# A fused attention and expert kernel: decay inverses by a backward scan, and one product as three products of high and low parts

## What is computed

```python
# r, k, v, w: (4, 8, 768, 48); u: (8, 48)
for t in range(S):                       # per batch and head
    y[t] = r[t] @ (state + outer(u * k[t], v[t]))
    state = w[t][:, None] * state + outer(k[t], v[t])
x = y as (3072, 384)
x = ((x @ w1) * (x @ w2)) @ w3 @ w_out   # w1, w2: 384x1024; w3: 1024x1024; w_out: 1024x384
# then a router (w_gate, w_noise, both 384x8) picks 2 of 8 experts for each token
out = sum over the two of weight * relu(x @ ew1[e]) @ ew2[e]
```

## Time and profile before

| | us |
|---|---|
| median of 3 runs | 982.52 |
| lowest and highest | 981.27, 983.54 |
| profiled execution, its own time | 980.96 |
| its span, first to last instruction | 979.2 |
| PE busy | 947.8 (97%) |
| DVE busy | 676.2 (69%) |
| ACT busy | 528.0 (54%) |
| L263, reciprocals, busy | 82.2 |

### The profile page before, as it was taken

The page is one execution under the profiler, slowest core; times in us unless marked ns, Lnnn a source line. Parts: engine busy times, 40 slices in busy tenths (PEclk is TensorE's granted clock), DMA queues, the critical chain, the costliest instruction groups (busy, mean ns, idle before and its releaser), DMA issues.

```text
span 979.2 us, 18038 instructions
## 1 busy us (share of the span) xinstructions
PE 947.8 (97%) x6825; PEld 894.3 (91%) x6825; DVE 676.2 (69%) x1133; ACT 528.0 (54%) x986; POOL 222.8 (23%) x209
## 2 busy tenths in 40 slices
PE   6989999999999999999989999999999999999995
PEld 4656999999999999999989999999999999999995
DVE  6997769888888875437766765757767468565570
ACT  4454445454555544326545665756657467565560
POOL 0000000202020111021453233333243332334321
PEclk9999999999999999999999999999999999999998
DMA  9996343544445121126557887877968779787751
GB/s 346 302 320 184 115 142 116 160 150 129 134 143 163 50 71 38 51 67 234 188 161 191 237 278 233 250 235 220 307 205 247 254 207 292 218 242 256 200 156 17
DMA packets 94347, 183.74 MB, mean 188 GB/s; under 512 B 18274, under 2 KB 49764, under 8 KB 94260
## 3 DMA queue, kind: packets, MB, share of 16 engines
q1 hardware_dynamic: 80884, 161.90, 50.8%
q0 software_dynamic: 12976, 20.66, 10.2%
q10 hardware_dynamic: 400, 0.02, 0.0%
HBM read 156.94 MB, written 26.97 MB: 188 GB/s over the span
## 4 chain that ended last, share of the span: by engine, by line
PE 87%; DVE 5%; ACT 3%; issue 2%; DMA 1%; SPq 0%; another core or an unknown queue 0%; POOL 0%; DVEq 0%; ACTq 0%; POOLq 0%
PE pp L1231 20%; PE bank L1215 20%; PE bank L786 13%; PE bank L803 7%; PE fx L786 6%; PE fx L803 4%; PE yu L1274 3%; PE pp L184 3%; PE tr L1196 2%; PE yu L1256 1%; PE fx L1256 1%; PE yu L205 1%; PE yu L235 1%; PE tr L193 1%; DVE kdiv L263 1%
## 5 line engine op out<-in xcount | busy, mean ns | idle before, releaser
L1125 POOL DMA_INDIRECT result<-x2s,who x55 | 92.5, 1681 | 290.3 <-ACT x2s L1348 277.4
L1335 DVE SCALAR_TENSOR_TENSOR abl<-bank,abh 128x512 fp32r<-128x512 f32 x96 | 66.2, 691 | 113.7 <-ACT abh L1330 97.5
L976 POOL DMA_INDIRECT slot_entry<-entry,slot_i x48 | 52.1, 1086 | 334.7 <-DVE token_f L965 322.5
L1215 PE MATMUL bank<-xh,set_up_h 128*128 128x256 f32 x384 | 109.2, 284 | 0.0
L1215 PE MATMUL bank<-xh,set_up_l 128*128 128x256 f32 x384 | 108.6, 283 | 0.0
L1215 PE MATMUL bank<-xl,set_up_h 128*128 128x256 f32 x384 | 108.6, 283 | 0.0
L1330 ACT ACTIVATE abh<-bank 128x512 fp32r<-128x512 f32 x96 | 57.5, 599 | 85.1 <-PE bank L1215 79.6
L786 PE MATMUL bank<-xh,w12h 128*128 128x384 f32 x264 | 89.5, 339 | 1.0 <-DVE xl L483 0.9
L786 PE MATMUL bank<-xh,w12l 128*128 128x384 f32 x264 | 88.4, 335 | 0.0
L786 PE MATMUL bank<-xl,w12h 128*128 128x384 f32 x264 | 88.2, 334 | 0.0
L1231 PE MATMUL pp<-set_down_h,abh 128*128 128x384 f32 x256 | 87.7, 342 | 0.0
(11 more groups left out here) (254 smaller groups left out, 2641.4 us busy)
## 6 DMA issues: line engine op xcount, KB each, us to landing
up_raw<-in_moe_w SPq DMA_DIRECT2D x93, 512.0 KB
down_raw<-in_moe_w SPq DMA_DIRECT2D x124, 384.0 KB
wt<-in_w SPq DMA_DIRECT2D x16, 384.0 KB, 3.2
kt<-in_k SPq DMA_DIRECT2D x16, 384.0 KB, 3.1
rt<-in_r SPq DMA_DIRECT2D x16, 384.0 KB, 3.6
vs<-in_v_rows SPq DMA_DIRECT2D x16, 384.0 KB, 3.7
kn<-in_k_rows SPq DMA_DIRECT2D x16, 288.0 KB, 3.2
rn<-in_r_rows SPq DMA_DIRECT2D x16, 288.0 KB, 3.6
```

The source lines that it names most:

```text
L976: nc.gpsimd.indirect_dma_start(slot_entry, bass.IndirectOffsetOnAxis(slot_i[:, s, n:n + 1], 0), entry[:, s, n, :], None).then_inc(scattere ...
L1125: nc.gpsimd.indirect_dma_start(out, bass.IndirectOffsetOnAxis(who[v % 4][:, s, 0:1], 0), yo[v % 2][:, s, 0:DM], None, bounds_check=N - 1, ...
L1215: last = nc.tensor.matmul(bank[m % 2][:, f * T2:(f + 1) * T2], wp[:, kk, c:c + P], xp[:, kk, :], start=(n == 0), stop=(n == 3 * KD - 1))
L1335: nc.vector.scalar_tensor_tensor(hl[:, 2 * m:2 * m + 2, :].rearrange("p a t -> p (a t)"), bank[m % 2][:, :], 0.0, hh[:, 2 * m:2 * m + 2, : ...
```

## The change

The inverse is made backward: one reciprocal of the last element of each of six chunks, then six scans over 127 elements from the end, each multiplying by the decay of the element behind. The load of the decays' input for the pair after next waits for these scans, since they read it, and SP issues it at derive 3, not 0.

Each product of w3 by the output weights becomes three float32r products. ACT makes the high parts (`woh` in two halves after wo_turn 2 and 5, its gate columns at gates_turn; `w3h` of block q + 1 at w3_mm q.1), DVE the low parts (`wol` at wo_gates and gates_turn, `w3l` of block q + 1 at w3_mm q.2), which overwrite the raw values. PE waits for `w3l_ready` where it waited for the load.

```diff
@@ sp_input_load
-            need(sp, (decay_ready, kdiv_ready, rdec_ready)[n], g - 1)
+            need(sp, (inverse_ready, kdiv_ready, rdec_ready)[n], (4, 1, 1)[n] * (g - 1))
@@ dve_inverse
-            two = slice(2 * third, 2 * third + 2)
-            nc.vector.reciprocal(kdiv[q % 2][:, :].rearrange("p (c x) -> p c x", c=NC)[:, two, :],
-                                 decay[q % 2][:, two, 1:C + 1]).then_inc(inverse_ready, 1)
+                nc.vector.reciprocal(kdiv[q % 2][:, :].rearrange("p (c x) -> p c x", c=NC)[:, :, C - 1:C],
+                                     decay[q % 2][:, :, C:C + 1]).then_inc(inverse_ready, 1)
+                dve.wait_ge(inverse_ready, 4 * g + 1)
+            for c in (2 * third, 2 * third + 1):
+                first, end = c * C, (c + 1) * C - 1
+                last = nc.vector.tensor_tensor_scan(backwards(kdiv[q % 2], first, end), backwards(wt[q % 2], first + 1, end + 1),
+                                                    backwards(wt[q % 2], first + 1, end + 1), kdiv[q % 2][:, end:end + 1],
+                                                    ALU.mult, ALU.bypass)
+            last.then_inc(inverse_ready, 1)
@@ sp_attention
-            elif step == "derive" and n in (0, 4, 5):
-                sp_input_load(sp, *after, max(0, n - 3))
+            elif step == "derive" and n >= 3:
+                sp_input_load(sp, *after, n - 3)
@@ first_act
+                def high(q):
+                    act.wait_ge(w3_loaded[q % 2], 16 * (q // 2 + 1))
+                    need(act, wa_full, q - 1)
+                    nc.scalar.copy(w3h[q % 2][:, :, :], w3T[q % 2][:, :, :]).then_inc(w3h_ready, 1)
...
                         evacuate(q)
+                        if q % KD == KD - 1:
+                            four = slice(4 * (q // KD), 4 * (q // KD) + 4)
+                            act.wait_ge(wo_loaded[q // KD], 16)
+                            nc.scalar.copy(woh[:, four, 0:DM], wo[:, four, 0:DM]).then_inc(woh_ready, 1)
...
+                        high(0)
+                    elif step == "gates_turn":
+                        act.wait_ge(gates_full, 2)
+                        nc.scalar.copy(woh[:, :, DM:WA].rearrange("p (j t) e -> p t j e", t=2), gate_columns).then_inc(woh_ready, 1)
+                    if step == "w3_mm" and n == 1 and q + 1 < KF:
+                        high(q + 1)
@@ first_dve
+                def lower_w3(q):
+                    dve.wait_ge(w3h_ready, q + 1)
+                    nc.vector.tensor_tensor(w3l[q % 2][:, :, :], w3T[q % 2][:, :, :], w3h[q % 2][:, :, :].bitcast(f32),
+                                            ALU.subtract).then_inc(w3l_ready, 1)
...
+                    if step == "wo_gates":
+                        for part in range(2):
+                            four = slice(4 * part, 4 * part + 4)
+                            dve.wait_ge(woh_ready, part + 1)
+                            dve.wait_ge(wb_full, KD * (part + 1))
+                            nc.vector.tensor_tensor(wol[:, four, 0:DM], wo[:, four, 0:DM], woh[:, four, 0:DM].bitcast(f32),
+                                                    ALU.subtract).then_inc(wo_ready, 1)
+                    elif step == "gates_turn":
+                        dve.wait_ge(woh_ready, 3)
+                        nc.vector.tensor_tensor(wol[:, :, DM:WA].rearrange("p (j t) e -> p t j e", t=2), gate_columns,
+                                                woh[:, :, DM:WA].rearrange("p (j t) e -> p t j e", t=2).bitcast(f32),
+                                                ALU.subtract).then_inc(wo_ready, 1)
+                        lower_w3(0)
+                    if step == "w3_mm" and n == 2 and q + 1 < KF:
+                        lower_w3(q + 1)
@@ first_pe
-                            pe.wait_ge(w3_loaded[q % 2], 16 * (q // 2 + 1))
-                            pe.wait_ge(wo_ready, 1)
+                            pe.wait_ge(w3l_ready, q + 1)
+                            pe.wait_ge(wo_ready, 3)
...
+                            for part, (wp, op) in enumerate(((w3h[q % 2], woh[:, m, :]), (w3h[q % 2], wol[:, m, :]),
+                                                             (w3l[q % 2], woh[:, m, :]))):
+                                last = nc.tensor.matmul(sums[q % 2][:, 0:WA], wp[:, m, :], op,
+                                                        start=(m == 0 and part == 0), stop=(m == KF - 1 and part == 2))
```

More of the change, by code:

```diff
@@ L254, in dve_decays, with backwards @@
             last.then_inc(decay_ready, 1)
+        def backwards(tile, first, end):
+            whole = tile[:, first:end]
+            (step, rows), _ = whole.ap
+            return bass.AP(whole.tensor, whole.offset + end - first - 1, [[step, rows], [-1, end - first]])
         def dve_inverse(dve, b, q, third):
@@ L502, in program @@
             gates_side = nc.alloc_sbuf_tensor_at("gates_side", [P, 2 * P], f32, offset=token_base + 4 * KD * F1)
+            w3_base = (nc.sbuf_base + 31) // 32 * 32
             w3T = [psb(f"w3T{i}", [P, KF, P]) for i in range(2)]
+            w3l = [nc.alloc_sbuf_tensor_at(f"w3l{i}", [P, KF, P], f32r, offset=w3_base + 4 * KF * P * i) for i in range(2)]
+            w3h = [nc.alloc_sbuf_tensor_at(f"w3h{i}", [P, KF, P], f32r, offset=token_base + 8 * TT * DM + 4 * KF * P * i) for i in range(2)]
+            woh = psb("woh", [P, KF, WA], f32r)
             pads = psb("pads", [P, PADS, WORDS], i32)
@@ L588, in first_act @@
                         nc.scalar.copy(gates_side[:, :], fx[:, 0:2 * P]).then_inc(gates_out, 1)
-                    elif step == "w3_mm" and n == 1 and 1 <= q <= 2 * KD:
+                        high(0)
[4 more added lines that the diff above has]
+                        high(q + 1)
+                    if step == "w3_mm" and n == 1 and 1 <= q <= 2 * KD:
                         m, kk = divmod(q - 1, KD)
@@ L626, in first_dve @@
                     dve_attention(dve, 0, step, q, n)
-                    if step == "gates_turn":
-                        dve.wait_ge(gates_full, 2)
-                        nc.vector.tensor_copy(wo[:, :, DM:WA].rearrange("p (j t) e -> p t j e", t=2),
-                                              fx[:, 2 * P:4 * P].rearrange("p (t j e) -> p t j e", t=2, j=4)[:, :, :, 0:2 * E]
-                                              ).then_inc(wo_ready, 1)
-                    elif step == "w3_mm" and n == 2 and 1 <= q <= 2 * KD:
+                    if step == "wo_gates":
[13 more added lines that the diff above has]
+                        lower_w3(q + 1)
+                    if step == "w3_mm" and n == 2 and 1 <= q <= 2 * KD:
                         m, kk = divmod(q - 1, KD)
@@ L675, in first_pe @@
                         if n == 0:
-                            pe.wait_ge(w3_loaded[q % 2], 16 * (q // 2 + 1))
-                            pe.wait_ge(wo_ready, 1)
+                            pe.wait_ge(w3l_ready, q + 1)
+                            pe.wait_ge(wo_ready, 3)
                             need(pe, wal_ready, q - 1)
                         for m in range(2 * n, 2 * n + 2):
-                            last = nc.tensor.matmul(sums[q % 2][:, 0:WA], w3T[q % 2][:, m, :], wo[:, m, :],
-                                                    start=(m == 0), stop=(m == KF - 1))
+                            for part, (wp, op) in enumerate(((w3h[q % 2], woh[:, m, :]), (w3h[q % 2], wol[:, m, :]),
+                                                             (w3l[q % 2], woh[:, m, :]))):
+                                last = nc.tensor.matmul(sums[q % 2][:, 0:WA], wp[:, m, :], op,
+                                                        start=(m == 0 and part == 0), stop=(m == KF - 1 and part == 2))
                         if n == 3:
```

6 lines of the change are left out of this document (5 added, 1 removed).

## The result

The changed kernel takes 1004.46 us (median; 1002.0 to 1007.48), the kernel before, run beside it, 982.36 (981.27 to 983.54). The ratio is 1.0224 [1.0203, 1.0246]: 22.1 us slower, about twice the 11.3 us that were forecast, and above the forecast range (984.5 to 1000.5). The profiled execution took 1007.48 us, the slowest of the four, with a span of 1005.8.

A forecast was written before the change was run, and what follows sets the result against it. DVE was taken to pace the first 93.7 us, PE the rest. The front's delay and the load waits, less savings, put the up products 11.3 us later: span 990.5, median 993.8 us, range 984.5 to 1000.5.

The forecast's parts named there:

- part 4: Loads of w3 blocks 2, 4 and 6, wanted sooner by casts: first masks +8.6, +13.3, +14.5 us; up products +11.3.
- What bounds the kernel: Up to 93.7 us DVE sets the pace, about 18 us a pair; behind that PE is full.
- Part 1: Inverse of the decays on DVE: one small reciprocal and six backward scans save 2.8 us a pair.
- Parts 2 and 3: w3's products save 8.1 us of PE, 0.26 a pair arriving; making the parts costs DVE 12.5 us.
- The front: Start up to the first mask: mask at 24.45 us instead of 18.21, pair 1's scans +7.6 us.
- Loads hidden: Rival, chance 0.15: w3 blocks land before the casts want them; +2.4 us, about 984.5.
- Slower still: Rival, chance 0.17: blocks land 2 to 2.5 us later or backward scans cost double; 5 to 8 more, about 1000.
- Faster: Rival, chance 0.08: PE sets the pace instead of DVE and its 8.1 us arrive; span down by 3 to 8.
- The change doesn't do what it says: Rival, counted in Slower still: backward scans cost what the reciprocals did; +5 us.

The follow-up runs named there:

- keep_warm_fitted: The changed kernel with idle products (12, 16, 18, none and 8) put into PE's waits: 999.93 us, ratio to the kernel before 1.0183.
- three_buffers: The changed kernel with a third w3 buffer, each block's load issued one block sooner: 983.78 us, ratio to the kernel before 1.0064.
- low_parts_on_pool: three_and_front with the low parts of w3 blocks 1 to 7 made on POOL, not DVE: 991.21 us, ratio to the kernel before 1.0136.
- three_and_front: three_buffers with the output weights' lower halves and the gate columns' cast moved later: 981.44 us, ratio to the kernel before 1.0039.

## Where the prediction was right, and where it failed

The direction and the mechanism held: the up products start late, the casts of blocks 2, 4 and 6 wait for a load, DVE stands behind them, and PE is full after that. The size was off by half: 993.8 us predicted and 1004.46 measured, 4 us above the range. The step that failed is part 4, the issue and the landing of the three loads and PE's clock around them.

**What bounds the kernel** held. DVE's busy time hardly changed, its idle time did, and from the end of the first 18 up products on the rest kept its length to 1.1 us.

**Part 1.** The reciprocals' 5.08 us became 0.19 for the small one and 2.35 for six scans. By form up to 140 us (count, busy us, mean ns, idle), the changed kernel:

```profile
L273 DVE TENSOR_TENSOR_SCAN kdiv<-wt,kdiv 128x127 f32<-128x127 f32 x36 | 15.0, 464 | 0.2
L252 DVE TENSOR_TENSOR_SCAN decay<-wt 128x128 f32<-128x128 f32 x36 | 12.0, 401 | 3.3 <-DMA wt<-in_w 3.3
```

A backward scan takes 464 ns, a forward one 401, so a pair saves 2.55 us (5.08 less 2.53) and not 2.8. The difference is hidden here, behind the waits for the casts.

**Parts 2 and 3** held: a quarter takes 1.1 us at the higher clock; the casts 1.04 us, the subtractions 1.21, the halves of the output weights 1.48 and 1.75.

**The front** held to half a us: first mask 24.45 predicted, 24.04 measured; pair 1's scans 30.7 and 30.91. PE was not idle from 17 us on, as the prediction had it, but only from 20.56, and still came back at the lower clock.

**Part 4** is the step that failed, term by term (all in us; masks, issues and the up products from the start of the span):

| | predicted | measured | added to the error |
|---|---|---|---|
| block 2 issued | 36.2 | 38.94 | +2.7 |
| pair 1's first mask | 44.6 | 47.87 | +0.5 |
| from there to block 4's issue | 14.6 | 16.9 | +2.3 |
| block 4, from issue to landing | 4.6 | 7.64 | +3.0 |
| from mask 2 to block 6's issue | 11.1 | 13.1 | +2.0 |
| block 6, from issue to landing | 5.1 | 4.12 | -1.0 |
| from mask 3 to the second mask | 1.9 | 2.8 | +0.9 |
| from there to the up products | 16.5 | 18.5 | +2.0 |
| up products start | 105.0 | 117.64 | +12.6 with rounding |

The first line: "the issue is tied to PE's progress" does not hold for block 2. PE had done block 0 at 36.8 us; the load went out at 38.94. It stands in SP's queue behind the loads of rows, which wait for DVE's product at 34.93 us, and behind the stores. The same stood in the kernel before (first DVE and SP before, then SP after):

```profile
26.84 0.70 DVE L287 TENSOR_TENSOR ruk<-kn,rn 128x576 f32<-128x576 f32 x1
...
27.56 0.33 SPq L152 DMA_DIRECT2D kn<-in_k_rows  x1
```

```profile
35.69 0.33 SPq L152 DMA_DIRECT2D kn<-in_k_rows  x1
```

From pair 1's scans to block 2's issue it is 7.80 us before, 8.03 after, and 8.05 in keep_warm_fitted, whose PE ran at the higher clock there. The prediction let it shrink to 5.5, since PE had less work.

The third line is the clock. "PE's work of pair 0 ... runs 2.0 us shorter (three quarters, two of which had run at the low clock)" and "less two shorter quarters" took it that the new quarters run at the higher clock. They ran at the lower one until 32.5 us (hidden there behind DVE), and so again from 46.9 to 56 (granted clock 0.50), from 79.7 to 84 and from 100.2 to 104 us. The prediction had priced the low clock for a single quarter, from the earlier trace rows, and then forgot it, though it had itself just put longer waits of PE in front of every block. With PE at the higher clock, in keep_warm_fitted, the third line takes 13.8 us. The two lines behind mask 3 fit the same cause: the second scores took 1.60 us instead of 0.94, and from the second mask to the store of the output it was 7.7 us instead of 5.7 before. The line from mask 2 to block 6's issue has two causes side by side, since keep_warm_fitted takes 12.9 us for it at the higher clock: there the copy of pair 2's output stands behind block 5's late cast. So of the 12.6 us 2.7 are DVE and SP's order ahead of block 2, some 5 the clock alone, 3.0 the store ahead of block 4, and 2.0 the clock or block 5's cast, either of them enough.

The landing of block 4 was copied from before, 4.6 us. The load now left SP 5.3 us after the big store (6.6 before) and took 7.64; with the store behind it, 4.46. How long a load takes to land depended on what stood beside it, and shifting the queue changes that.

"Blocks 3, 5 and 7 are wanted later in the pair and cost no wait" was wrong for 5 and 7, though in the changed kernel it cost little. ACT's lines in order of time, changed kernel:

```profile
84.15 1.05 ACT L605 CAST w3h<-w3T 128x1024 fp32r<-128x1024 f32 x1 [2.41 <-DMA w3T<-in_moe_w]
...
104.47 1.04 ACT L605 CAST w3h<-w3T 128x1024 fp32r<-128x1024 f32 x1 [2.21 <-DMA w3T<-in_moe_w]
...
106.36 0.47 ACT L370 COPY yt<-yu 128x384 f32<-128x384 f32 x1
```

PE's product that this copy waits for:

```profile
105.26 0.88 PE L235 MATMUL yu<-att,vs 128*64 128x128 f32 x12
```

What stands behind a waiting cast in ACT's queue is the copy of a pair's output. Behind block 7's it is that of the last pair (106.36), and so the stores of the output (from 106.86), the load of the first group of tokens that waits for them (issued at 111.51, landed at 116.46) and the up products. But PE, at the lower clock, had that output ready only at 106.14, so that the cast's wait added 0.2 us at most, and block 5's 0.4 (ready at 85.64, copied at 86.05). The prediction named DVE behind the cast, never the copy.

The last 2.7 us of the profiled span come after the up products have begun: the first 18 took 4.96 us and not 3.40, at a granted clock of 0.66; the other 1.1 I didn't follow. In the profiles the growth is 26.6 us, on the medians 22.1: this execution was the slowest of its four, and the one profiled before (980.96) faster than all of its own.

**The price of a load.** The load of 512 KB took 4.1 to 7.6 us where the chain passes through it. The Trainium skill (DMA: Bandwidth & Descriptors, Anatomy of one DMA; Bandwidth) would make it an estimated 3.2 us, which the prediction rounded to 3.3; its figures are for loads that GpSimd issues, where SP issues these, and no run here shows them. With such loads part 4's chain gets up to 4.9 us shorter (1.8, 1.3 and 1.8), not the "about 3" of the prediction. With the issue one block earlier the loss fell from 22 to 6 us; that agrees with the rule of the Trainium skill (DMA: Bandwidth & Descriptors, Rules for kernel authors) to issue early and wait late.

**The rivals.** Loads hidden (+2.4) is what three_buffers makes true by force, and it measures +6.3 [4.1, 8.4]: no cast waits, and still 4 us more than worked out, with 27.2 us at the lower clock. Slower still was right in its sign, and named late landings and a dearer scan; what it lacked was that PE's waits bring back the lower clock, and this delays the next issue. *Faster* was far off: the first mask came at 24.04 us, where it wanted less than 21. *The change doesn't do what it says* had the scans' failing to pay, for another reason than the one given: they are cheap and their gain has nowhere to go.

**What is left open.** The low clock's price is bounded from below only; no run with the three products kept PE at 2.4 GHz all through. The parts don't add up: the load waits (16 us), the front (2.5 to 3.3), the pads' store (5) and the clock (5) overlap, and each was measured by taking it away from the whole.

## What to carry to other kernels

A step that reads a loaded buffer sooner than its old reader takes lead from the load, and the load's issue has to move with it. Look up the time between issue and first use of every block in the old trace, subtract what the new reader takes away, and compare with the slowest landing, not the usual one; where the issue follows the consumer's progress, each wait is passed on to the next block and can grow. Read from the trace what each issue really waits for: a queue that is worked off in order can tie a load to an engine that never touches it.

When a queue gets a new wait, list all that stands behind it in that queue, the small copies too. And a cheaper instruction and an earlier load can each be worth nothing alone and 7 us together.

## What the runs showed of the hardware that was not expected

While POOL ran a subtraction with two operands in SBUF, DVE's instructions with two operands in SBUF stood still. A 128x1024 subtraction takes POOL 2.42 us and DVE 1.21. The six scans beside it took 4.18 us instead of 1.99: one of them 2.61, the others 0.39 each. By form up to 107 us, low_parts_on_pool and then three_and_front:

```profile
L252 DVE TENSOR_TENSOR_SCAN decay<-wt 128x128 f32<-128x128 f32 x30 | 18.6, 690 | 3.5 <-DMA wt<-in_w 3.5
L656 POOL TENSOR_TENSOR w3l<-w3T,w3h 128x1024 fp32r<-128x1024 f32 x7 | 17.0, 2424 | 75.7 <-ACT w3h L611 75.7
...
L694 DVE TENSOR_TENSOR w12l<-wraw,w12h 128x1024 fp32r<-128x1024 f32 x6 | 9.9, 1656 | 2.6 <-ACT w12h L634 2.6
```

```profile
L252 DVE TENSOR_TENSOR_SCAN decay<-wt 128x128 f32<-128x128 f32 x36 | 12.0, 402 | 3.3 <-DMA wt<-in_w 3.3
...
L692 DVE TENSOR_TENSOR w12l<-wraw,w12h 128x1024 fp32r<-128x1024 f32 x6 | 7.3, 1218 | 0.0
```

The Trainium skill (SBUF — State Buffer, SBUF: two separate sides) states that the two engines take their shared pair of ports by an exclusive lock, for a whole instruction, and the trace agrees: of POOL's 17.0 us 13.4 are missing on DVE, spread over all seven subtractions. The rest fell before DVE's next such instruction had begun. The busy time of an instruction on DVE then includes its wait, as in the scan of 2.61 us.

A scan that runs backwards and starts from a value in SBUF costs 464 ns for 127 elements, against 401 ns for a forward one of 128. Which of the two makes the difference was not told apart.

The record of TensorE's clock missed a stretch: one execution shows 1.00 where the products stand 0.333 us apart, another of the same kernel 0.50 at the same place. Where the clock carries an argument, the spacing of equal products is the surer sign.
